# Reordering the first loads of a fused attention and feed-forward kernel, and moving the centroids' norms behind two weight tiles

## What is computed

```
c_n = centroids / (norm(centroids) + 1e-6)
q_assign, k_assign = argmax(q_n @ c_n.T), argmax(k_n @ c_n.T)
scores = where(q_assign == k_assign, q @ k.T / 8, -1e9)
x = softmax(scores) @ v                      # 1536 x 512
x = ((x @ w1) * (x @ w2)) @ w3 @ w_out       # d_ff 1024
h = x @ w_in;  y = (h * clip(h + 3, 0, 6) / 6) @ w_out2   # d_ff 2048
```

## Time and profile before

| | us |
|---|---|
| median of 3 runs | 713.5 (713.37 to 713.72) |
| the profiled execution, its own time | 715.35 |
| its span, first to last instruction | 713.5 |
| PE busy | 705.0 (99%) |
| POOL, DVE, ACT busy | 446.5, 496.1, 390.9 |
| granted TensorE clock, mean | 1.000 |

### The profile page before, as it was taken

One profiled execution on the slowest core, in us unless ns is written; L12 is line 12 of the kernel. 1 busy time (PEld: TensorE's weight loads), 2 busy tenths in 40 slices (PEclk: granted clock), 3 DMA queues, 4 the chain that ended last, 5 costly groups with the idle time before them and its releaser, 6 DMA issues.

```text
span 713.5 us, 11831 instructions
## 1 busy us (share of the span) xinstructions
PE 705.0 (99%) x4017; PEld 607.4 (85%) x4017; DVE 496.1 (70%) x754; ACT 390.9 (55%) x808; POOL 446.5 (63%) x455
## 2 busy tenths in 40 slices
PE   8998999999999999999999999999999999999998
PEld 6787777776767767999999999999988889998886
DVE  6237787877878786677986779888865547874221
ACT  6315565656656575454554445477754447775333
POOL 5953553453354475996969969788557769753221
PEclk9999999999999999999999999999999999999999
DMA  8647765665565413211002110012212233221212
GB/s 294 188 105 201 185 124 133 162 162 139 142 168 125 111 23 71 71 65 55 15 16 86 64 60 1 30 60 89 75 47 73 74 102 120 74 76 60 69 35 90
DMA packets 41772, 68.50 MB, mean 96 GB/s; under 512 B 10224, under 2 KB 17904, under 8 KB 41712
## 3 DMA queue, kind: packets, MB, share of 16 engines
q1 hardware_dynamic: 36048, 64.81, 32.2%
q10 hardware_dynamic: 5664, 2.93, 1.4%
HBM read 44.07 MB, written 3.19 MB: 66 GB/s over the span
## 4 chain that ended last, share of the span: by engine, by line
PE 93%; issue 2%; DVE 2%; ACT 1%; POOL 1%; DMA 1%; SPq 0%; POOLq 0%
PE ps L1377 21%; PE ps L1379 21%; PE ps L1378 21%; PE ps L1503 9%; PE ps L1489 8%; PE ps L1477 5%; PE ps L1479 4%; PE ps L1446 1%; DMA wo_raw<-in_wo 1%; DVE g_lo L1295 1%; ACT probs L799 0%; PE ps L1463 0%; PE ps L1408 0%; PE ps L1411 0%; DVE neg_max L1159 0%
## 5 line engine op out<-in xcount | busy, mean ns | idle before, releaser
L634 POOL TENSOR_TENSOR b_lo<-stage,b_hi 128x512 fp32r<-128x512 f32 x94 | 111.9, 1191 | 101.3 <-ACT b_hi L882 101.1
L1295 DVE TENSOR_TENSOR g_lo<-gate,g_hi 128x384 fp32r<-128x384 f32 x96 | 83.6, 878 | 64.9 <-ACT g_hi L971 64.8
L799 ACT ACTIVATE probs<-ps,neg_max 128x768 f32<-128x768 f32 x96 | 86.8, 904 | 51.4 <-DVE neg_max L1159 50.6
L1159 DVE TENSOR_REDUCE neg_max<-ps 128x1 f32<-128x768 f32 x96 | 91.2, 952 | 25.1 <-PE ps L1479 24.9
L971 ACT CAST g_hi<-gate 128x384 fp32r<-128x384 f32 x96 | 49.2, 514 | 90.4 <-PE ps L1379 90.4
L1489 PE MATMUL ps<-ident,probs 128*128 128x128 f32 x576 | 77.6, 275 | 0.0
L1489 PEld LDWEIGHTS ps<-ident,probs 128*128 128x128 f32 x576 | 66.1, 140 | 13.4 <-ACT probs L799 7.2
L1220 DVE COPY probs_t<-ps 128x512 f32<-128x512 f32 x96 | 63.7, 679 | 17.3 <-PE ps L1489 17.1
L591 POOL TENSOR_TENSOR x_lo<-x_raw,x_hi 128x384 fp32r<-128x384 f32 x15 | 15.2, 1016 | 96.7 <-PE ps L1489 64.4
L1180 DVE TENSOR_TENSOR sum_lo<-sum_raw,sum_hi 128x768 fp32r<-128x768 f32 x64 | 65.2, 1021 | 14.5 <-ACT sum_hi L858 14.3
L1379 PE MATMUL ps<-b_hi,g_lo 128*128 128x512 f32 x192 | 74.8, 389 | 0.0
(11 more groups left out here) (129 smaller groups left out, 1846.7 us busy)
## 6 DMA issues: line engine op xcount, KB each, us to landing
stage<-in_wio SPq DMA_DIRECT2D x64, 256.0 KB, 2.6
qk_ops<-qk_split SPq DMA_DIRECT2D x32, 384.0 KB, 5.8
stage<-in_w SPq DMA_DIRECT2D x46, 256.0 KB, 3.1
qk_raw<-in_qk SPq DMA_DIRECT2D x16, 384.0 KB, 5.2
qk_ops<-qk_split SPq DMA_DIRECT2D x32, 192.0 KB, 5.7
v_raw<-in_v SPq DMA_DIRECT2D x16, 192.0 KB, 2.6
recip_all<-recip_rows SPq DMA_DIRECT2D x32, 96.0 KB, 3.1
out<-out_sb ACTq DMA_DIRECT2D x11, 256.0 KB, 2.2
```

The lines of the kernel that those rows point to most:

```text
L634: nc.gpsimd.tensor_tensor(b_lo[n % 2][:, cols], stage[n % 2][:, cols], b_hi[n % 2][:, cols].bitcast(F32), ALU.subtract).then_inc(s_lo[half ...
L799: nc.scalar.activation(probs[g % PROBS][:].rearrange("p (a b) -> p a b", a=2), scores[g % 2], ACT.Exp, bias=neg_max[:, g:g + 1], scale=1.0 ...
L1159: nc.vector.tensor_reduce(neg_max[:, g:g + 1], scores[g % 2], AX.XY, ALU.max, negate=True).then_inc(s_max, 1)
L1295: nc.vector.tensor_tensor(g_lo[i][:], hidden(q, c, f)[0][:], g_hi[i][:].bitcast(F32), ALU.subtract).then_inc(s_glo, 1)
```

## The change

On SP, wo's tiles 0 and 1 come first, then the two rests, then the centroids; the two pieces are issued by ACT, ahead of all its other work. On ACT the square root moves behind the cast of wo's tile 1. On DVE the low part of wo's tile 0 comes ahead of the centroids' squares, and that of tile 1 between the sum of squares and the rest of the norm.

```
@@ sync
-            def load_piece(n):
-                sp.dma_start(stage[n][:, PIECE], w3[n][:, PIECE]).then_inc(s_piece[n], 16)
-            sp.dma_start(cent_raw[:], cent).then_inc(s_cent, 16)
-            load_piece(0)
-            load_wo(0)
-            load_piece(1)
-            load_wo(1)
+            load_wo(0, 1)
             load_rest(0)
             load_rest(1)
+            sp.dma_start(cent_raw[:], cent).then_inc(s_cent, 16)
             load_wo(2, 3)
@@ scalar
-            act.wait_ge(s_cent_sq, 1)
-            nc.scalar.activation(cs[1][:], cs[0][:], ACT.Sqrt).then_inc(s_sqrt, 1)
+            for n in range(2):
+                act.dma_start(stage[n][:, PIECE], w3[n][:, PIECE]).then_inc(s_piece[n], 16)
             piece_high(0)
             wo_high(0)
             piece_high(1)
             wo_high(1)
+            act.wait_ge(s_cent_sq, 1)
+            nc.scalar.activation(cs[1][:], cs[0][:], ACT.Sqrt).then_inc(s_sqrt, 1)
             rest_high(0)
             rest_high(1)
             wo_high(2)
@@ vector
+            wo_low(0)
             dve.wait_ge(s_cent, 16)
             step(nc.vector.tensor_tensor(cent_sq[:], cent_raw[:], cent_raw[:], ALU.mult))
             own.wait()
             nc.vector.tensor_reduce(cs[0][:], cent_sq[:], AX.X, ALU.add).then_inc(s_cent_sq, 1)
+            wo_low(1)
             dve.wait_ge(s_cent_sq, 1)
             dve.wait_ge(s_sqrt, 1)
...
-            for k in range(F1T):
+            for k in range(2, F1T):
                 wo_low(k)
```

## The result

| | before | after |
|---|---|---|
| median of the runs, us | 713.61 (713.37 to 714.00, 4 runs) | 719.78 (718.35 to 720.57, 4 runs) |
| ratio, with 95% interval | | 1.0078 (1.0057 to 1.0099) |
| profiled execution, own time | 715.35 | 719.89 |
| its span | 713.5 | 718.1 |
| first matmul of the fold's block 2 | 18.56 | 24.68 |

The account below looks back on a forecast made before the run. PE, busy 99% of the span, bounds the kernel, so step 2's L1411 start decides: L + 4.61 = 10.48 us, unchanged. A small wait at 14.07 goes, -0.08, giving 713.4 us from a 713.5 median; range 712.7 to 714.8.

Parts of the forecast that it names:

- SP's order: SP's queue: wo's tile 2 is issued at 3.06 us instead of 3.99, 0.93 earlier, and so is all behind it.
- the middle case: Loads at the front: work queued sooner fills the DMA engines' idle share, 0.93 us, so wo's tile 1 lands at 5.87.
- L: Time when wo's tile 1 lands: bounded by 5.40 and 6.67 us, taken as 5.87; 6.80 before.
- the sum: Path through ACT and DVE to PE's L1411 pair of step 2: L + 4.61 = 10.48 us, same as before.
- A: Loads at the front land much sooner, L near 5.4 or less: -0.55, 712.9 us; chance 0.20.
- B: Wo's tile 1 lands hardly sooner, L = 6.67: +0.80 - 0.08, 714.2 us; chance 0.22.
- ACT's table load: On ACT, between the cast of wo's tile 1 and the square root: a second table load, 1.28 + 0.03 us.
- Rival D: The table load empties ACT first, adding a stop of 1.28 us once more: 714.7 us; chance 0.05.
- rival C: Centroids, now SP's fifth load, come too late; landing with wo's tile 2 at 8.12 gives 714.3 us; chance 0.10.
- the norm's chain from 3.39 to 4.97, so 1.58: On DVE, behind the square root and ahead of wo's tile 2's low part: the norm takes 1.58 us, as before.
- Low part beside POOL: DVE's low part of wo's tile 2: taken as 0.69 us, with +0.62 beside POOL's L550 kept for the range.
- I let the front's difference pass through whole: PE's stall at 67.31 us moves along with PE, so the front's difference reaches the end.

Follow-up runs that it names:

- e4: Changed kernel, with POOL's subtractions for the second halves of w3's blocks 0 and 1 waiting until the norm is done: 720.44 us, ratio 1.0096.
- e6: Changed kernel's loads, with square root behind ACT's last cast of wo, norm behind DVE's last low part, transpose later: 713.91 us, ratio 0.9999.
- e2: Changed kernel with SP's load order and the pieces as before, so only the norm's new place remains: 717.31 us, ratio 1.0043.
- e7: Changed kernel, with POOL's two scalings of qk waiting until DVE has made all eight low parts of wo: 719.08 us, ratio 1.0071.
- e5: Changed kernel, with ten identity matmuls ahead of PE's wait in step 2: 719.51 us, ratio 1.0076.
- e9: Changed kernel with the edits of e5 and e7 together: 717.07 us, ratio 1.0027.
- e1: Kernel before, with wo's tiles ahead of the rests and pieces on ACT's queue; centroids still first, norm in its old place: 713.98 us, ratio 1.0005.
- e8: e1 with POOL's scalings waiting for the last low part of wo, as in e7: 713.25 us, ratio 0.9982.
- e10: Changed kernel with e3's dummy square root at ACT's head and the POOL waits of e4 and e7: 714.78 us, ratio 0.9997.
- e11: The same kernel as e8, timed once more: 714.75 us, ratio 0.9998.
- e3: Changed kernel with one dummy square root at ACT's head, so its table is loaded there and not between the casts: 717.43 us, ratio 1.0031.
- e12: The kernel of e8 and e11 with ten identity matmuls at PE's start instead of eight: 713.61 us, ratio 0.9984.

## Why the prediction was wrong

**SP's order and the queues: right in kind, a little off in size.** The idle DMA share was filled, as taken for the middle case. But the pieces on ACT's queue were cast 4.1 us (0.73 to 4.79) and 4.7 us (1.17 to 5.87) after their issue, where I had taken 2.4 from before as the least. Wo's tile 1 was there when its turn came, since its cast at 6.18 waited for no DMA; it stood behind the second piece's cast, and L became 6.18 in effect: +0.31. Wo's tile 2 was cast at 8.82; the sum had 8.87. Rivals A and B fall.

**ACT's table load: right.** It starts 0.02 after the cast ahead and the root 0.01 after its end. Rival D falls: 6.82 + 1.28 + 0.01 = 8.11.

**Centroids (rival C): not late.** DVE squared them at 6.67 without waiting, and the root followed the table load.

**The step that failed is "DVE": "the norm's chain from 3.39 to 4.97, so 1.58".** I carried the price of the chain from a place where it hardly meets POOL to one where POOL works almost without a gap. It measured 4.69. This term alone is +3.11 of the 3.29 by which step 2 was late. The old place, which I called an idle stretch, is not quite that:

```profile
4.02 0.72 POOL L599 TENSOR_TENSOR b_lo<-stage,b_hi 128x256 fp32r<-128x256 f32 x1 [2.57 <-ACT b_hi L818]
```

This operation stands beside the one-input operations L1121 and L1123, which take 0.15 and 0.16, and ends at 4.74, 0.06 before the first scaling does. So the old price was taken where no operation had POOL in its way for long.

I had asked what POOL does to the low part, and kept 0.62 for it, but not what POOL does to the eight operations ahead of it; I also saw POOL's L550 pair move forward, from 11.07 to "near 10.8", and booked it as a gain of 0.08. It came at 10.55, on top of the scaling. That the scaling's price is POOL's is shown by e4 (0.25 each again once POOL waits). That the place costs the time is shown by e6, where moving it takes all of the loss away, and by e2, where it alone costs 0.43%.

The Trainium skill (SBUF — State Buffer, "SBUF: two separate sides") says that DVE and GpSimd share one pair of SBUF ports, that a DVE operation in a two-port mode or with two SBUF inputs and a GpSimd operation exclude one another for a whole instruction, and that the loser blocks. That is the rule that spoke against this change, and it was not among those I weighed. The traces agree in kind: the column products with two inputs grew from 0.16 to 0.62, one-input column operations kept 0.15 and 0.16 beside POOL (e6), and copies out of PSUM (L1133) took 0.27 to 0.29 beside POOL, the same as in e7, where the first stands mostly ahead of POOL's row. Which mode the scaling of the centroids runs in, no trace shows; that it is blocked, they do.

**"Low part beside POOL": the range kept 0.62, the runs showed more.** The six low parts from tile 2 on took 10.42 us, one of them 4.60. I took my bound from the mean of four, 1.31, in which single ones took up to 1.78; and the trace of before has no low part beside POOL's scaling of q (L562, from 18.05), since the last one ends at 16.92. This term was to move step 2 alone. I had also said that PE is continuous from step 2's L1411 pair on, so that this pair is the number to forecast. With low parts this long it was not: the chain ends in tile 6's low part at 22.28.

**The clock was no term at all.** I took a late step as an addition of its length. Behind a wait of 2.5 us PE ran at 1.2 GHz from 13.4 to 16.7, which moved its next pairs by 1.40 us more. By e5, e7 and e9 this loss and the 4.60 us operation overlap: neither removal alone moves block 2 by more than 0.2 us, both together by 2.7.

**"I let the front's difference pass through whole".** In the profiled executions 6.12 us at block 2 became 4.6 in the span. From block 2 to the end before has 694.9 us, the longest of all, and after 693.4; in it PE waits 1.69 us for POOL's scaling at 67.31. Here is that stretch of after, where the long waits are these two:

```profile
70.10 0.62 PE L1475 MATMUL ps<-qk_ops 128*128 128x384 f32 x2 [0.53 <-ACT probs L793]
...
73.75 0.66 PE L1487 MATMUL ps<-ident,probs 128*128 128x128 f32 x4 [0.32 <-DVE probs_t L1218]
```

That stall does not move along with PE, as I had it from the one trace. It is 1.38 us in e2 and 1.56 in e6, 0.50 to 0.80 in e1, e4, e8, e10 and e11, and absent in after, e3, e5, e7, e9 and e12. Before's profiled execution was also 1.7 us above the median of its timed runs. If most of those lack the stall, the medians' 6.17 us are the front's 6.12 passing through whole; but no trace of such a run exists, and two of after's four runs have a mean clock of 0.995 where the profiled one has 0.998. This stays open.

The likeliest case had 0.43 and its relatives most of the rest: none of the rivals A to D had an operation that grows in its new place. The range was built from shifts of 0.1 to 0.9 us in landings; the loss came from durations that I had treated as fixed.

## What to carry to other kernels

An instruction's duration belongs to the place where it was measured. Before moving a chain of small DVE operations, lay POOL's timeline beside the new place, at the times that the change itself gives it. Price each operation with two SBUF inputs, and each scaling of a whole tile (128 x 64 here) from SBUF to SBUF, at the end of the POOL operation beside it, and do the same for the operations behind the chain, to the last one that PE needs. Allow for a stretch at half clock behind a long wait of PE: waits of 2.50, 2.82 and 3.52 us brought one (after, e4, e7), one of 2.62 did not (e5). And expect that removing one of several overlapping delays shows nothing.

## What the hardware did that I had not expected

- A DVE operation can stay blocked over a whole row of POOL operations: 4.60, 4.57 and 4.57 us for a low part of 0.69 (after, e4, e5) and 4.19 for a scaling of 0.25 (e6), each time beside the same four POOL operations without a gap: two L556, the scaling of q, and two L544. It ends 0.05 to 0.55 us after the last of them. The Trainium skill (SBUF — State Buffer, "SBUF: two separate sides") has the loser blocked for a whole instruction; here it was four. Elsewhere, beside L544 or L550 alone, the two engines took turns, with low parts of about 1.77 each. What decides between taking turns and being held is open; e7 shows only that the hold goes when L556 and what follows it wait.
- The half clock came and lasted differently: 3.4 us of it after 2.50 and 2.82 us of idle time (after, e4), 6.8 us after 3.52 (e7), none after 2.62 (e5). At the front too it varied: by the lengths of its pairs PE was at full speed from about 6.6 in e7 and from about 9.9 in after, with idle times of 0.48 and 0.47 us ahead of step 0. The runs do not say why.
- A table load in the middle of ACT's work (after, 6.82) cost its 1.28 us and 0.03 beside it, nothing more. The Trainium skill (ScalarE: Activation LUTs, "What ACT_TABLE_LOAD costs") has the same length for the load, and a drain on top that no trace here shows.
- With the pieces on a second queue the DMA engines' share rose (0.92 and 1.05 for 0.73 and 0.74), but a piece took longer from issue to cast: 4.1 and 4.7 us, against 2.4 for the first piece on SP's queue before.
